# First feed-forward layer as three fp32r products from split parts of w_in that are streamed from memory for each block, with the early loads in another order

## What is computed

```python
scores = q @ k^T / 8                     # batch 2, heads 8, 576 x 576, head width 64
scores = where(scores >= 32nd largest of the row, scores, -1e9)
x = softmax(scores) @ v                  # then laid out as 1152 tokens x 512
h = x @ w_in                             # 512 -> 2048: the layer of this change
g = maximum(h, 0) + alpha * minimum(h, 0)
x2 = g @ w_out                           # 2048 -> 512
out = top-2-of-8 mixture: relu(x2 @ w1[e]) @ w2[e], weighted
```

## Time and profile before

| | |
|---|---|
| median of three runs | 770.1 us (767.59 to 772.91) |
| the profiled execution, its own time | 770.31 us |
| its span, first to last instruction | 768.6 us |
| mean granted TensorE clock | 0.958 of full speed |
| busy: PE, PEld | 683.8 us (89%), 534.7 us (70%) |
| busy: DVE, ACT, POOL | 511.7 (67%), 462.5 (60%), 377.7 us (49%) |
| L870, first layer, in two groups | 124.4 and 7.2 us busy |
| L901, second layer, in two groups | 100.1 and 56.9 us busy |
| moved by DMA | 98.89 MB, mean 129 GB/s |

### The profile page before, as it was taken

One profiled execution on the slowest core, in us unless ns is written; L12 is line 12 of the kernel. 1 busy time (PEld: TensorE's weight loads), 2 busy tenths in 40 slices (PEclk: granted clock), 3 DMA queues, 4 the chain that ended last, 5 costly groups with the idle time before them and its releaser, 6 DMA issues.

```text
span 768.6 us, 13559 instructions
## 1 busy us (share of the span) xinstructions
PE 683.8 (89%) x4516; PEld 534.7 (70%) x4516; DVE 511.7 (67%) x1092; ACT 462.5 (60%) x878; POOL 377.7 (49%) x429
## 2 busy tenths in 40 slices
PE   2456999999889999999999989649999999999993
PEld 2345567767567667667677656449989989989992
DVE  5998998787777888888888223754555555545520
ACT  5786767777968677777676644813544544545511
POOL 3558787767866766667767745400202202202112
PEclk9975899999999999999999999859999999999998
DMA  9287023222114141040440263271539358366222
GB/s 323 122 326 285 15 57 134 97 88 76 59 32 140 72 144 37 1 165 14 151 151 1 95 223 125 106 256 59 149 140 286 105 183 259 92 223 209 82 33 35
DMA packets 36720, 98.89 MB, mean 129 GB/s; under 512 B 10480, under 2 KB 11504, under 8 KB 35184
## 3 DMA queue, kind: packets, MB, share of 16 engines
q1 hardware_dynamic: 32288, 88.31, 32.8%
q0 software_dynamic: 4384, 9.98, 5.8%
HBM read 80.15 MB, written 37.34 MB: 153 GB/s over the span
## 4 chain that ended last, share of the span: by engine, by line
PE 75%; ACT 7%; POOL 6%; issue 4%; DMA 3%; DVE 3%; SPq 0%; ACTq 0%; POOLq 0%; DVEq 0%
PE bank L870 13%; PE bank L901 13%; PE bank L1055 11%; PE ps_scores L1041 9%; PE bank L1041 6%; PE bank L852 6%; PE ps_scores L797 4%; PE bank L1060 4%; PE bank L836 3%; DMA q_raw<-q_rows_dram 2%; PE bank L882 2%; POOL expo L1488 2%; PE bank L1023 1%; POOL k_parts L1445 1%; DVE top L383 1%
## 5 line engine op out<-in xcount | busy, mean ns | idle before, releaser
L383 DVE MAX8 top<-rest 128x8 f32<-128x576 f32 x216 | 152.3, 747 | 0.0
L1616 POOL DMA_INDIRECT out_dram<-ye,xe x24 | 42.8, 1783 | 217.3 <-ACT ye L1396 212.4
L1488 POOL TENSOR_TENSOR expo<-scores,expo 128x576 f32<-128x576 f32 x72 | 101.8, 1415 | 92.7 <-ACT scores L1123 92.6
L870 PE MATMUL bank<-w_in_sb,x_t 128*128 128x512 f32 x272 | 124.4, 600 | 0.0
L391 DVE MATCH_REPLACE8 rest<-top,rest 128x576 f32<-128x576 f32 x144 | 105.9, 743 | 0.0
L901 PE MATMUL bank<-w_out_high,g_parts 128*128 128x512 f32 x288 | 100.1, 410 | 0.0
L383 DVE MAX8 top<-scores 128x8 f32<-128x576 f32 x72 | 53.8, 752 | 64.3 <-ACT scores L1092 42.2
L1055 PE MATMUL bank<-w_hi,he_t 128*128 128x512 f32 x256 | 91.9, 400 | 0.0
L565 DVE TENSOR_TENSOR w_lo<-raw,w_hi 128x1024 fp32r<-128x1024 f32 x64 | 77.9, 1225 | 19.4 <-ACT w_hi L1338 18.4
L870 PEld LDWEIGHTS bank<-w_in_sb,x_t 128*128 128x128 f32 x272 | 49.9, 191 | 50.3 <-issue 49.6
L852 PEld LDWEIGHTS bank<-v,prob_t 128*64 128x64 f32 (+1 forms) x1440 | 56.8, 144 | 38.2 <-issue 18.0
(11 more groups left out here) (188 smaller groups left out, 1489.6 us busy)
## 6 DMA issues: line engine op xcount, KB each, us to landing
raw<-w_dram SPq DMA_DIRECT2D x64, 512.0 KB, 9.1
x_sorted_dram<-x_sorted_dram SPq DMA_DIRECT2D x7, 2570.0 KB, 10.5
q_raw<-q_rows_dram SPq DMA_DIRECT2D x18, 256.0 KB, 2.7
xe<-x_sorted_dram SPq DMA_DIRECT2D x8, 514.0 KB, 4.3
w_out_raw<-w_out_dram SPq DMA_DIRECT2D x4, 1024.0 KB, 12.2
w_in_sb<-w_in_dram SPq DMA_DIRECT2D x4, 1024.0 KB, 8.8
out_dram<-x_now SPq DMA_DIRECT2D x1, 3584.0 KB, 28.1
x_sorted_dram<-x_now SPq DMA_DIRECT2D x1, 2570.0 KB, 18.9
```

What stands on the lines that cost most here:

```text
L383: nc.vector.max(dst, src).then_inc(chain if r < ROUNDS - 1 else dve_top, 1)
L870: mm = pe.matmul(dst, x_t[:, k, :], w_in_sb[:, k, c * 512:(c + 1) * 512], start=(k == 0), stop=(k == MK - 1))
L1488: nc.gpsimd.tensor_tensor(expo[:, n % 4, :], scores[:, n % SBUFS, :], expo[:, n % 4, :], ALU.mult).then_inc(pool_prob, 1)
```

## The change

**First layer.** x_t is kept as a high and a low fp32r part, w_in too. `first_layer` is now twelve fp32r matmuls: for each of the four k, high x with high w_in and with low w_in, and after these eight, low x with high w_in. For c = 0 the last four wait for the low part of x.

**Low part of x.** VectorE makes it (`low_x`), straight from PSUM, after pair 2 of the block.

**w_in.** Only two chunks (of four) fit at a time, in `w_in_parts`. In the ramp each chunk (1 MB) is loaded, split (`high_w_in` on ScalarE, `low_w_in` on GpSimd, eight pieces each) and its two parts (2 MB) are written to memory. From block j = 1 on, each `first_layer(j, c)` reads its chunk back (`next_w_in`), which may start once `first_layer` of the chunk before last is done.

**Smaller edits.** `neg` has one buffer instead of two, so `relu_both` also waits for the `prelu` before it. The last block's gates read from `x2_t` instead of `x_t`. SP's loop over the last blocks is written out.

```diff
-W_HIGH_AT = {2 + c: c for c in range(8)}
-W_LOW_AT = {5 + c: c for c in range(8)}
+W_HIGH_AT = {4: 0, 5: 1, 6: 2, 7: 3, 8: 4, 9: 5, 14: 6, 15: 7}
+W_LOW_AT = {6: 0, 7: 1, 8: 2, 9: 3, 10: 4, 11: 5, 16: 6, 17: 7}
+W_IN_HIGH_AT = {0: (0,), 1: (1,), 2: (2,), 3: (3,), 11: (4, 5), 13: (6, 7)}
+W_IN_LOW_AT = {2: 0, 3: 1, 4: 2, 5: 3, 12: 4, 13: 5, 14: 6, 15: 7}
...
+            def low_x(j):
+                dve.wait_ge(act_xt, j + 1)
+                nc.vector.tensor_tensor(x_t[:, 1, :, :].rearrange("p k n -> p (k n)"), ps_t[:, :],
+                                        x_t[:, 0, :, :].rearrange("p k n -> p (k n)").bitcast(F32),
+                                        ALU.subtract).then_inc(dve_xt, 1)
...
+                    if pair == 2 and not first:
+                        low_x(blk - 1)
...
+            def load_w_in(c):
+                if c > 1:
+                    sp.wait_ge(pe_first, c - 1)
+                    sp.wait_ge(w_in_stored[c - 2], 16)
+                sp.dma_start(w_in_raw[:, c % 2, 1, :], w_in[:, c * MK * 512:(c + 1) * MK * 512]).then_inc(w_in_in[c], 16)
+            def next_w_in(j, c):
+                sp.wait_ge(pe_first, 4 * j + c - 1)
+                if j == 1:
+                    sp.wait_ge(w_in_stored[c], 16)
+                    if c < 2:
+                        sp.wait_ge(w_in_stored[c + 2], 16)
+                sp.dma_start(w_in_parts[:, c % 2].rearrange("p a n -> p (a n)").bitcast(F32), w_parts[c]).then_inc(w_in_back[c % 2], 16)
...
+                if isinstance(j, int) and j == 0:
+                    pe.wait_ge(pool_w_in_low, 2 * c + 2)
+                else:
+                    pe.wait_ge(w_in_back[c % 2], 32 * j - 16 + 16 * (c // 2))
...
                 for k in range(MK):
-                    mm = pe.matmul(dst, x_t[:, k, :], w_in_sb[:, k, c * 512:(c + 1) * 512],
-                                   start=(k == 0), stop=(k == MK - 1))
+                    for b in range(2):
+                        pe.matmul(dst, x_t[:, 0, k, :], w_in_parts[:, c % 2, b, k * 512:(k + 1) * 512],
+                                  start=(k == 0 and b == 0), stop=False)
+                if c == 0:
+                    pe.wait_ge(dve_xt, j + 1)
+                for k in range(MK):
+                    mm = pe.matmul(dst, x_t[:, 1, k, :], w_in_parts[:, c % 2, 0, k * 512:(k + 1) * 512],
+                                   start=False, stop=(k == MK - 1))
...
             sp.wait_ge(x2_stored, 16 * EARLY)
             sp.dma_start(x2[:, 0:EARLY, 0:MODEL], x2_rows[:, :, :].rearrange("b p n -> p b n")).then_inc(x2_back, 16)
+            next_w_in(BLOCKS - 1, 2)
+            next_w_in(BLOCKS - 1, 3)
```

More of the change, by code:

```diff
@@ L444, in _ @@
             row_sums(BLOCKS - 1, 1)
+            low_x(BLOCKS - 1)
             steps = [0]
@@ L1118, in high_w_out, with high_w_in @@
                 nc.scalar.copy(w_out_high[:, at], w_out_raw[:, at]).then_inc(act_w_high, 1)
+            def high_w_in(piece):
+                c, lo = piece // 2, MK * 256 * (piece % 2)
+                act.wait_ge(w_in_in[c], 16)
+                nc.scalar.copy(w_in_parts[:, c % 2, 0, lo:lo + MK * 256],
+                               w_in_raw[:, c % 2, 1, lo:lo + MK * 256]).then_inc(act_w_in_high, 1)
             def sign_tile(tile, n, pairs):
@@ L1173, in copy_x_t @@
                 wait(act, pe_first, 4 * j)
[L1174 removed]
+                nc.scalar.copy(x_t[:, 0, :, :].rearrange("p k n -> p (k n)"), ps_t[:, :]).then_inc(act_xt, 1)
             def copy_h1(j, c):
@@ L1281, in one_block @@
                         exp_tile(tile + 3, h + 3, PAIRS * blk + (h + 2) // 2 + 1)
+                    for piece in W_IN_HIGH_AT.get(tile, ()) if isinstance(tile, int) else ():
+                        high_w_in(piece)
                     if isinstance(tile, int) and tile in W_HIGH_AT:
```

129 lines of the change are left out of this document (88 added, 41 removed).

## The result

The changed kernel takes 796.3 us (median of 4 runs, 795.4 to 797.6), the kernel before 770.3 on the same chip: 1.034 times as long, with a 95% interval of 1.030 to 1.038. The prediction said 785, between 773 and 796. The direction was right, the loss was 26 us instead of 15.

A forecast was written before the change was run, and what follows sets the result against it. TensorE was taken to bound the steady blocks. +3.9 (blocks 2, 4 to 8) + 2.7 (block 3) + 4.5 (block 1) - 1.3 (tail) + 5 (clock) = +14.8 us on 770.31 gave 785 us, range 773 to 796.

The forecast's parts named there:

- The saving: TensorE's 36 first layers: each takes 2.88 us instead of 3.52, saving 0.64 us, 2.56 us a block.
- The stall: TensorE at c = 0 waits for low x behind VectorE's pair 2: 3.2 us a block, 4.0 in block 3.
- the loop argument: TensorE's wait for low x returns every block: the loop takes 13.43 us, with only 10.22 us of TensorE work.
- The clock: TensorE's clock may fall behind stalls in blocks 2 to 8: 0.7 us for each of seven, +5 us.
- The third rival: Every stall pays for the clock in full, 7 x 1.3 = 9.1 us instead of 5: 789, band 788 to 793; chance 0.13.
- The ramp and blocks 1 and 2: GpSimd's `low_w_in` pieces delay first layers in block 1, +4.5 us; block 2 stalls for low x, +0.65 before clock.
- Block 3: Stall of 4.0 us less two first-layer savings of 0.64, as only c = 0 and 1 are on the chain: +2.7 us.
- The tail: Last block's first layers save 2.56 us, the last chunk landing late costs 1.2: -1.3 us.
- The stream hidden: Reading w_in chunks back, 8 MB a block, 8 us per 2 MB chunk, costs zero, hidden by four tiles.
- the single buffer free: One buffer of `neg` costs nothing, as GpSimd runs `prelu` at the tile's start, before ScalarE's next ReLU.

The follow-up runs named there:

- stall_filled: Changed kernel with eight products of high x and low w_in repeated twice at c = 0, before the wait for low x; 784.9 us.
- low_x_in_pair: Changed kernel with VectorE's subtraction for low x ahead of the third round of pair 2 instead of behind the whole pair; 762.4 us.
- tail_raw_behind_chunk: Changed kernel with SyncE waiting for the last w_in chunk to land before issuing the loads of the first expert's weights; 799.1 us.
- ramp_low_on_vector: Changed kernel with pieces 4 to 7 of `low_w_in` made on VectorE instead of GpSimd; 793.8 us.
- x2_load_behind_chunks: low_x_in_pair plus ramp_low_on_vector, with `first_layer(8, 1)` right behind `first_layer(8, 0)` and x2's load issued behind the last two w_in chunks; 761.5 us.

## Why the prediction was right and where it was not

- **The saving (0.64 us a first layer, 2.56 a block)**: right. Without the stall a steady block takes 43.3 us against 46.0, 2.7 less.
- **The stall (3.2 us, 4.0 in block 3)**: right in place and in cause. It recurs in each block, as the loop argument had it. In size it is right in blocks 4 to 8: 2.8 to 3.3 us idle, and 3.2 us between stall_filled and low_x_in_pair. In blocks 2 and 3 it was 1.9 and 2.2 us, and 3.3 and 4.0 had been put.
- **The clock (0.7 us a stall)**: the step that failed in the steady blocks. A stall of 2.9 us is followed by a fall in all of blocks 4 to 8 of the changed kernel, and a fall costs 1.6 us there (stall_filled, and block 5 of tail_raw_behind_chunk, the one such stall with no fall behind it). I had set the price midway between one stretch where the clock stayed and one where it fell; both the chance of a fall and its price, 1.3 at most, were put too low. -2.7 + 3.2 + 1.6 = +2.1 us is what blocks 5 to 8 show, against 1.35 forecast: 2.8 us of the miss. The third rival had this, with 1.3 us each. The rule of the Trainium skill cited there, "TensorE: Matmul & The Clock Gate", section "A second HAM failure mode: psum-queue depth-cycling", points the right way, and the trace agrees: up and down once in each of blocks 4 to 8.
- **The ramp and blocks 1 and 2 (+4.5 and, with its clock, +1.35)**: +6.0 and +0.1, together 0.3 more than forecast, in part by luck: in block 2 the stall was 1.4 us shorter than put and no clock was lost. The marks came as worked out: c = 0 done at 83.1 us (83.4 forecast, though the low part came 0.4 us later and the four products took 1.2 us, not the 1.8 of the lower clock), c = 2 started at 101.8 (101.5), c = 3 at 115.3 (115.0), x of block 1 at 126.9 ("about 126"). That last delay did lie inside the stall of block 2, which came out at 1.88 us instead of 3.3, and there the clock did not fall (in tail_raw_behind_chunk, the same program up to the tail, it was 2.46 us and the clock fell). What was missing is the stall of block 1 as a cost: I compared its end with the kernel before and found it no later. Both causes lie in the same stretch, and taking one away alone gives back 4.5 us (low_x_in_pair) or 4.1 (ramp_low_on_vector).
- **Block 3 (+3.4 with its clock)**: +5.5. Here too the term that failed is the clock. The windows of the whole block, before, of the change, of low_x_in_pair and of x2_load_behind_chunks:

```profile
167.03:224.44 57.41, 51.52 (x368) 37.33 (x369) 40.58 (x85) 45.56 (x90) 41.73 (x47) 0.97 0.17 51
173.19:236.14 62.95, 53.45 (x384) 43.60 (x385) 41.30 (x86) 45.53 (x90) 41.72 (x47) 0.89 0.55 204
167.76:226.69 58.93, 51.63 (x384) 42.50 (x385) 41.13 (x86) 45.48 (x90) 41.76 (x47) 0.91 0.58 215
165.26:221.47 56.21, 48.93 (x384) 40.13 (x385) 41.18 (x86) 45.50 (x90) 41.86 (x47) 0.97 0.61 227
```

Without the stall the block takes 56.2 and 56.3 us in the two whole kernels whose mean clock is 0.97, as before, and 58.8 to 59.3 in the three with 0.91. So at the same clock the faster products give 1.2 us, as counted (1.3). The stall with its clock gave back 4.0 (low_x_in_pair), where 4.7 had been put. The miss is that the changed kernel's block has a clock of 0.89 instead of 0.97, more than one fall behind one stall: some falls stand behind other waits of the block, such as the one of 2.1 us for scores, and low_x_in_pair keeps them. Why some profiles have them and others not is open.
- **The tail (-1.3)**: +3.5, the largest single miss, 4.8 us. The step that failed was the landing time of the last chunk: 8 us after its issue, by the earlier trace rows and their 7.7 us for the x2 load. That load had the queues nearly to itself; in the tail of the changed kernel it stands in front of both chunks and takes 13.1 us. The last chunk took 11.1 us, TensorE stood idle 4.3 us, not 1.2, and then ran eight products in 3.46 us instead of 2.1. The saving of 2.56 us was right: without the stream the tail is 2.7 us shorter than before (21.5 against 24.2).
- **The stream hidden, the single buffer free**: no wait for a chunk outside the tail, and blocks 4 to 8 do not change when the stream is left out. That the buffer of `neg` costs nothing was not tried by itself; 43.3 us for a block with TensorE never idle leaves no room for it there.

The misses add up: 0.3 (blocks 1 and 2) + 2.1 (block 3) + 0.3 (block 4) + 2.8 (blocks 5 to 8) + 4.8 (tail) = 10.3 us, and 25.1 - 14.8 is 10.3. So two steps failed: the clock (blocks 3 to 8, 5.2 us) and the landing time of the last chunk (4.8 us).

## What to carry to other kernels

When one operand of a matmul group is made late, price the wait as idle time plus the clock behind it, and look first for an earlier place on the engine that makes it: here a low part of x that is ready 4.0 us earlier in the block turned a loss of 3.4% into a gain of 1.1%. If no earlier place exists, needed work moved into the gap should be worth more than its own length, since even repeated products there saved 1.6 us a block; such a move was not run. And take a transfer's landing time from a stretch in which the queues are as full, not from a quiet one.
